# Rank-32 mixing in a fused attention and MLP kernel: the sums of x as six products in 128x64 tiles, and span scores of both tiles ahead of the global ones

## The reference

```
scores = scale * q @ k.T + bias; scores = where(keep, scores, -1e9); a = softmax(scores); x = a @ v
xt = x.transpose(0, 2, 1)
h = xt @ U @ V                       # U: 768 x 32, V: 32 x 768
u = x + h.transpose(0, 2, 1)
u = u + max(u @ w_ch1, 0) @ w_ch2    # 512 -> 2048 -> 512
xk, xr = blends of u and u one position earlier
out = sigmoid(xr @ w_r) * (max(xk @ w_k, 0) ** 2 @ w_v)
```

## Time and profile before

| | |
|---|---|
| median of 3 runs | 524.52 us (522.78 to 524.78) |
| profiled execution, its own time | 522.44 us |
| its span in the trace | 520.7 us |
| PE busy | 508.3 us, 98% |
| DVE, ACT, POOL busy | 184.3, 131.1, 243.4 us |
| PE records in the sums of x (L471) | 192, mean 277 ns |
| granted TensorE clock | 0.999 of full |

### The profile page before, as it was taken

How to read it: one execution, slowest core, us unless ns; L and a number is a source line. 1 busy time by engine, 2 the same in 40 slices (tenths; PEclk the granted TensorE clock), 3 DMA queues, 4 the chain that set the end, 5 groups by cost and what they waited for, 6 DMA issues and landing times.

```text
span 520.7 us, 9725 instructions
## 1 busy us (share of the span) xinstructions
PE 508.3 (98%) x3824; PEld 423.7 (81%) x3824; DVE 184.3 (35%) x479; ACT 131.1 (25%) x352; POOL 243.4 (47%) x228
## 2 busy tenths in 40 slices
PE   4899999999999999999999999999999999999997
PEld 3788888888888888888888888888888888888885
DVE  5777775121313313133131331312443233441323
ACT  4777775101100011000110001121322132213220
POOL 3254657165008100079700729990899579960000
PEclk9999999999999999999999999999999999999999
DMA  6876755204002200024400000000000200020002
GB/s 213 284 242 229 226 189 162 81 0 162 0 0 70 92 0 0 0 66 162 157 20 0 0 0 0 1 0 1 0 1 0 81 0 0 0 81 0 0 0 81
DMA packets 15344, 33.84 MB, mean 65 GB/s; under 512 B 1488, under 2 KB 1872, under 8 KB 15312
## 3 DMA queue, kind: packets, MB, share of 16 engines
q1 hardware_dynamic: 14736, 32.57, 18.5%
q10 hardware_dynamic: 576, 0.84, 0.5%
HBM read 30.25 MB, written 3.15 MB: 64 GB/s over the span
## 4 chain that ended last, share of the span: by engine, by line
PE 97%; DVE 1%; DMA 1%; issue 1%; POOL 0%; ACTq 0%; POOLq 0%
PE psum L582 25%; PE psum L570 25%; PE psum L635 13%; PE psum L626 13%; PE psum L650 6%; PE psum L429 5%; PE psum L441 4%; PE psum L463 3%; PE psum L455 1%; PE psum L471 1%; PE psum L481 1%; PE psum L478 1%; DMA k_in<-in_k 1%; PE psum L479 1%; DVE probs L863 0%
## 5 line engine op out<-in xcount | busy, mean ns | idle before, releaser
L978 DVE SCALAR_TENSOR_TENSOR HL<-psum,HH 128x512 fp32r<-128x512 f32 x48 | 33.2, 692 | 171.9 <-ACT HH L762 171.9
L762 ACT ACTIVATE HH<-psum 128x512 fp32r<-128x512 f32 x48 | 28.8, 600 | 229.3 <-PE psum L570 229.3
L582 PE MATMUL psum<-HH,w2h 128*128 128x512 f32 x192 | 75.0, 391 | 0.0
L570 PE MATMUL psum<-UH,w1h 128*128 (+1 forms) x192 | 74.8, 389 | 0.1
L582 PE MATMUL psum<-HL,w2h 128*128 128x512 f32 x192 | 74.7, 389 | 0.0
L582 PE MATMUL psum<-HH,w2l 128*128 128x512 f32 x192 | 74.7, 389 | 0.0
L570 PE MATMUL psum<-UH,w1l 128*128 (+1 forms) x192 | 74.7, 389 | 0.0
L570 PE MATMUL psum<-UL,w1h 128*128 (+1 forms) x192 | 74.7, 389 | 0.0
L1100 POOL TENSOR_SCALAR w1h<-raw 128x2048 fp32r<-128x2048 f32 x4 | 7.7, 1919 | 118.0 <-PE psum L582 118.0
L1017 DVE TENSOR_TENSOR k_square<-k_relu 128x512 f32<-128x512 f32 x24 | 24.2, 1010 | 66.3 <-ACT k_relu L787 66.2
L681 ACT ACTIVATE probs<-probs,neg_max 128x192 f32<-128x192 f32 x96 | 42.5, 444 | 19.8 <-DVE neg_max L863 19.8
(11 more groups left out here) (118 smaller groups left out, 883.2 us busy)
## 6 DMA issues: line engine op xcount, KB each, us to landing
v_in<-in_v SPq DMA_DIRECT2D x16, 384.0 KB, 4.4
raw<-in_moe_w_ch SPq DMA_DIRECT2D x6, 1024.0 KB, 5.1
v_rest<-in_v_rest SPq DMA_DIRECT2D x8, 384.0 KB, 3.7
out<-result SPq DMA_DIRECT2D x12, 256.0 KB, 2.0
k_in<-in_k SPq DMA_DIRECT2D x7, 432.0 KB, 3.9
q_in<-in_q SPq DMA_DIRECT2D x7, 384.0 KB, 3.1
raw<-in_moe_w_ch SPq DMA_DIRECT2D x8, 256.0 KB, 4.3
raw<-in_moe_w_v SPq DMA_DIRECT2D x2, 1024.0 KB, 5.1
```

Of the source, the lines that this page charges most:

```text
L570: mm = pe.matmul(bank[4 + f % 2][:, 0:BLK], w[:, kt, f * P:(f + 1) * P], x[:, kt, ds(blk * BLK, BLK)], start=kt == 0 and n == 0, stop=kt = ...
L582: mm = pe.matmul(bank[d][:, 0:BLK], w[:, f, d * P:(d + 1) * P], x[:, f % 2, :], start=f == 0 and n == 0, stop=f == FQ - 1 and n == 2)
L762: act.activation(HH[:, f % 2, :], bank[4 + f % 2][:, 0:BLK], ACT.Relu).then_inc(hid_high, 1)
L978: dve.scalar_tensor_tensor(out=HL[:, f % 2, :], in0=bank[4 + f % 2][:, 0:BLK], scalar=0.0, in1=HH[:, f % 2, :].bitcast(F32), op0=ALU.max, ...
```

## The change

`U` is laid out twice side by side (64 columns in place of 32), and its tile moves from beside `x_nat` to behind `probs_t`. The sums of x are six products, one per position tile, each 64 columns wide, in place of twelve that are 32 wide. Even tiles go to partitions 0 to 63, odd tiles to 64 to 127. High and low rows of `A4` now alternate (high 0 to 31 and 64 to 95, low 32 to 63 and 96 to 127), so `a_low` subtracts in two instructions of 32 partitions, and `a_ready` counts to 2 for each pair. V stands four times over as before. In `scores` the loops are exchanged: the span products of both tiles come first, then the global ones.

```diff
@@
-        U = region("U", [P, ST, RANK])
@@
+        U = region("U", [P, ST, 2 * RANK])
@@ def scores(n):
-                for i, t in unit_tiles(n):
-                    for frm, w, to in ((t * P, SPAN, i * (WIN + GLOB)), (None, GLOB, SPAN + i * GLOB)):
+                for w in (SPAN, GLOB):
+                    for i, t in unit_tiles(n):
+                        to = i * (WIN + GLOB) if w == SPAN else SPAN + i * GLOB
                         for j in range(GROUPS):
                             for h in range(2):
                                 r = slice(h * D, (h + 1) * D)
-                                k_at = BAND if frm is None else frm + j * GROUP
+                                k_at = t * P + j * GROUP if w == SPAN else BAND
@@ def sums_of_x(x):
                 for t in range(ST):
-                    for side in (t % 2, t % 2 + 2):
-                        mm = pe.matmul(bank[M_BANK][side * RANK:(side + 1) * RANK, 0:P], U[:, t, :], x(t),
-                                       start=t < 2, stop=t >= ST - 2)
+                    side = t % 2
+                    mm = pe.matmul(bank[M_BANK][side * 2 * RANK:(side + 1) * 2 * RANK, 0:P], U[:, t, :], x(t),
+                                   start=t < 2, stop=t >= ST - 2)
@@ def mixing(p, part):
-                    pe.wait_ge(a_ready, p + 1)
+                    pe.wait_ge(a_ready, 2 * p + 2)
@@ def a_low(p):
-                r = slice(2 * RANK, 4 * RANK)
-                dve.tensor_tensor(A4[r, p % 2, :], bank[M_BANK][r, 0:P], A4[r, p % 2, :].bitcast(F32),
-                                  ALU.subtract).then_inc(a_ready, 1)
+                for side in range(2):
+                    r = slice((2 * side + 1) * RANK, (2 * side + 2) * RANK)
+                    dve.tensor_tensor(A4[r, p % 2, :], bank[M_BANK][r, 0:P], A4[r, p % 2, :].bitcast(F32),
+                                      ALU.subtract).then_inc(a_ready, 1)
```

More of the change, by code:

```diff
@@ L37, in block_kernel @@
     DM = H * D
-    RANK = mix_u.shape[2]
+    RANK = mix_u.shape[2] // 2
     BH = B * H
@@ L1217 @@
     laid["counts"] = laid["counts"].astype(np.int64).view(np.int32)
-    laid["moe_U"] = inputs["moe_U"].reshape(tiles, P, -1).transpose(1, 0, 2)
+    laid["moe_U"] = np.tile(inputs["moe_U"].reshape(tiles, P, -1).transpose(1, 0, 2), (1, 1, 2))
     laid["moe_V"] = np.tile(inputs["moe_V"], (4, 1))
```

## The result

The changed kernel takes 525.35 us (median of 21 executions) against 522.29 us for the kernel before (21 executions): ratio 1.0058, 95% interval 1.0042 to 1.0073, so 3.06 us or 0.58% slower. Measured again, beside other kernels, it was 524.58 against 522.33 us, ratio 1.0040 (1.0018 to 1.0062). Three executions far above all others (639.72 and 979.9 us, with mean granted clocks of 0.758 and 0.895, and 1786.04 us of the kernel before) are in no ratio. The time forecast, 525.4 us, was met, but partly by offset: its base of 523.6 us was 1.3 too high and its step of +1.8 us 0.5 to 1.3 too low. That the time came out to a tenth of a microsecond is luck.

A forecast was written before the change was run, and what follows sets the result against it. In six of eight pairs the path was taken to run from scores through DVE and ACT to a_low and PE's L478, with PE's stream otherwise. 1.92 - 0.10 = +1.8 us on 523.6 gave 525.4 us, range 522.9 to 527.8.

The forecast's parts named there:

- its base of 523.6 us: Time of the kernel before, taken as the mean of the known executions at 522.4, 522.8, 524.5 and 524.8 us.
- its step of +1.8 us: Whole kernel: 1.92 us for the split subtraction less 0.10 us for pair 6.
- The second subtraction: DVE's a_low: second half starts 0.32 us behind the first, on the path in pairs 0 to 5, +1.92 us.
- PE's saving: Sums of x on PE: 0.66 us in place of 0.79, 0.13 us less per pair, hidden in pairs 0 to 5.
- Pair 6: The one pair where PE's shorter sums count, up to the later end of a_low: minus 0.1 us.
- Rival 1: Time lost between PE's shapes is on the path, the second subtraction is not: -0.9 us, 522.7 us, chance 0.08.
- Scores and U: The new score order and the doubled load of U in the fill were each taken as worth 0.
- rival 2: Narrow scores in a row run at 0.03 us each: -2.9, in sum -1.1 us, 522.5 us, chance 0.07.
- rival 3: Narrow scores in a row starve for weights, 0.09 for 0.06 us: in sum +4.7 us, 528.3 us, chance 0.07.
- rival 4: The sums' two 128x64 parts take turns, 1.32 us in place of 0.79: +3.8 us, 527.4 us, chance 0.04.
- rival 5: The subtraction's halves overlap wholly on DVE, a_low ends at most 0.1 us later: +0.5 us, 524.1 us, chance 0.12.
- the forecast's own range of 1.2 to 2.0 us: Range of the slowdown if the forecast itself holds, which was given a chance of 0.62.

The follow-up runs named there:

- run 1: The kernel before with only a_low split into two subtractions of 32 partitions; 526.0 us, ratio 1.0107.
- run 10: The changed kernel with ACT's copy of the sums moved between the two exponents of the first head; 522.17 us, ratio 1.0005.
- run 7: The kernel before with the first half of a pair's mixing placed behind the scores on PE, ACT's copy for it moved likewise; 524.07 us, ratio 1.0019.
- run 8: The changed kernel with one masked subtraction over 128 partitions and the first half of the mixing behind the scores; 523.68 us, ratio 1.0026.
- run 9: The kernel before with ACT's copy of the sums between the two exponents of the first head; 521.73 us, ratio 0.9984.
- run 11: The changed kernel with one masked subtraction over 128 partitions and ACT's copy of the sums between the two exponents; 521.49 us, ratio 0.9987.
- run 3: The changed kernel with the scores in their old order, span and global products alternating by tile; 525.74 us, ratio 1.0061.
- run 2: The kernel before with U laid out twice and moved, the sums still twelve products of 32 columns; 522.17 us, ratio 1.0003.
- run 5: The kernel before with 15 more DVE instructions in the branch that is never taken; 523.55 us, ratio 1.0036.
- run 6: The changed kernel without the subtraction in the branch that is never taken; 523.4 us, ratio 1.0015.
- run 12: The changed kernel itself, measured again beside the early-copy kernels; 524.58 us, ratio 1.0040.
- the masked kernels: The three kernels, run 4, run 8 and run 11, with a_low as one masked subtraction over 128 partitions; ratios 1.0023, 1.0026 and 0.9987.
- run 4: The changed kernel with a_low as one masked subtraction over all 128 partitions; 522.58 us, ratio 1.0023.

## Why the prediction was right, and what it left out

**The second subtraction: right in mechanism and size.** The forecast gave a step of 0.32 us and +1.92 us over six pairs, on the path in full. The step is 0.32 us, the period went from 9.98 to 10.30, and run 1 reproduces this with nothing else changed. Run 10 shows the cause by moving the chain 0.44 us earlier with the same two instructions in place: PE's wait falls to some 0.1 us and the period to 9.86.

**PE's saving: right in sum, wrong in its parts.** The forecast was 0.13 us per pair, as sums of 0.66 us. The sums take 0.71 us (59.06 less 58.35), and L464 gives back the rest: 0.56 us to the transposes (59.62 less 59.06), where L463 took 0.62. Together it is 0.14. That it is hidden in pairs 0 to 5 was right, and runs 7 and 8 and runs 9 and 11 bring it out, 0.14 and 0.13 us. Pair 6, where it was to count by 0.10, gained 0.14: from pair 5's first mixing product to pair 6's is 9.49 us after (90.84 less 81.35) and 9.63 before (86.53 less 76.90). The rule of "TensorEngine Tiling (Array Packing)", Key Properties, in the Trainium skill, that a change of tiling mode drains the engine, agrees with these rows; run 7, with two more changes of mode in a round and 0.33 us more, is the plainest. Rival 1, which put the saving on the path and not the subtraction, fell with the period.

**Scores and U: right.** First score to L456 stayed at 0.80 us and run 3 equals the changed kernel, so rivals 2 and 3 fell; U twice as wide is worth nothing (run 2). The two parts of 128x64 run side by side, so rival 4 fell, and the halves of the subtraction don't overlap, so rival 5 fell.

**What the sum left out is the end of the program.** It took the attention as "the only stage that the change touches", and the tail is 0.9 us longer. With it the sum is 1.92 - 0.13 + 0.92 = +2.7 us, inside both measured intervals (2.2 to 3.8 and 0.9 to 3.2 us), where +1.8 is under the first, and the forecast's own range of 1.2 to 2.0 us holds neither of the measured steps, 3.06 and 2.25. So of the 1.3 us by which the step was too low at the first measurement, 0.9 lie here.

This also moved the result to the edge of what the prediction called telling: slower by over 0.5% had a chance of 0.11, by rivals 3 and 4. The first measurement, 0.58% (0.42 to 0.73), is there by neither of them, and the second, 0.40%, is under it.

The cause of the longer tail is the length of DVE's program, by experiment: 15 unused instructions bring it on (run 5), and leaving 14 out takes it away (run 6). An eleventh instruction packet and the long tail came together in runs 1, 3, 5, 10 and 12, and in the seven others there was neither. How the packet delays the store is seen only in part: it lies at 523.6 to 523.8 us among the last store's packets, and when all others have landed, five packets of that store still come one by one between 524.5 and 524.9, as from one DMA engine that has fallen behind. That last part is a reading, not shown. The Trainium skill ("Runtime: NRT & Kernel Launch", Instruction fetch mechanics) says of crossing a block boundary in the program that its cost is mostly hidden. For DVE itself that holds here (run 5's period stays at 9.98 us); for a store whose landing ends the program it was 0.9 us.

**Do the times bear the sum out?** In part. Executions with a mean granted clock under 0.998 are among the longest (the next paragraph shows where one of them lost its clock), so I leave them out on both sides. The means then differ from the kernel before by 2.6 us in run 12, 0.9 in run 5, 0.1 in run 10 and -0.9 in run 11. Period, pair 6, tail, and the 0.3 us of the masked kernels add up to 2.7, 0.9, 0.1 and -1.0. Runs 1, 4 and 6 fit less well: 3.8 us (four executions) for 2.9, 1.0 for 0.5, and 1.2 for 1.8.

**What stays open: the first 26 us.** In the profiled execution of the changed kernel the first mixing product of pair 0 is at 29.83 us and in run 12 at 28.31, where it was at 26.75; only 0.32 us of that is the subtraction. In eleven of the fourteen traces PE stops between two groups of the same L455 product (L456 after the change), with no releaser: for 1.30 us before, 1.91 after, 2.18 in run 12, and 0.81 to 1.91 in the others. In runs 4, 5 and 9 it doesn't stop. A 16 KB instruction packet of q8 starts 2.2 to 2.5 us ahead of the end of each stop (before: 16.64 and 18.94 us; after: 18.25 and 20.49). In the three traces without a stop it starts 3.1 to 3.6 us ahead of the start of the same product. So a late fetch of PE's program fits all fourteen traces, but no experiment moved the fetch alone. A stop of 0 to 2.2 us is as large as most of what single executions of one kernel differ by; that it is the reason is not shown. In the profiled execution there is something more. Windows of 12 to 20 and 20 to 26 us of it, and 20 to 26 of run 12 (the number behind the last engine is the granted clock):

```profile
12.00:20.00 8.00, 6.07 (x146) 5.27 (x143) 5.54 (x32) 6.60 (x28) 2.66 (x2) 1.00 0.99 333
20.00:26.00 6.00, 5.51 (x101) 4.79 (x101) 2.26 (x12) 2.14 (x10) 0.91 (x1) 0.72 0.38 131
```

```profile
20.00:26.00 6.00, 5.59 (x152) 4.91 (x153) 3.52 (x15) 3.32 (x14) 0.91 (x1) 1.00 0.59 211
```

Behind the stop, from 20.46 us on, PE ran for 3.4 us at 1.2 in place of 2.4 GHz, which makes the mean 0.72; six transposes took 1.54 us, not 0.87. From the product's second part to the next round's L456 it is 3.99 us (24.48 less 20.49), where it was 2.53 before (21.47 less 18.94), so the lower clock cost some 1.5 of the 2.3 us by which this execution is above the median. Runs 3 and 6, with stops of 1.84 and 1.91 us, show the same fall. Run 12 stopped for longer and kept its clock, so the length of the stop alone doesn't decide it. The changed kernel's executions fall apart the same way: four with a mean clock of 0.997 took 527.6 to 527.8 us, fifteen with 0.998 or more took 523.5 to 526.7.

## What to carry to other kernels

Price an edit on the chain that ends last, not on the engine that looks busiest: the saving of 0.13 us per pair was real and hidden, the 0.32 us on a small engine was on the path, and moving one copy by 0.44 us in a third engine's queue took 0.44 us per pair off the changed kernel, more than either. Where an instruction is split, look first for one that does all partitions with a mask: here it cost 0.06 us per pair in place of 0.32. And compare the tail and the count of instruction packets before explaining half a per cent by executed work, since code that never runs can move the end of the program.

## What was not expected of the hardware

- 15 instructions that are never executed lengthened the program's end by 0.9 us (4.2 in place of 3.2), with one 8 KB instruction packet more (11 in place of 10). How the packet holds up the last store is not shown.
- Two subtractions of 32 partitions in disjoint rows don't overlap on DVE: 0.61 us for two of 0.29. Over 128 partitions the masked form takes 0.35.
- One more excursion from 64x64 to 128x128 tiles and back costs PE 0.33 us in a round (run 7).
- The stop of PE in the fill falls at the same instruction, behind 6 of 16 records of L455, in kernels with old and new sums alike. It lasts 0.8 to 2.2 us where it shows, in eleven of fourteen traces, and ends 2.2 to 2.5 us behind the start of a 16 KB instruction packet.
- PE's granted clock fell to half for 3.4 us behind stops of 1.84, 1.91 and 1.91 us (runs 3 and 6, and the changed kernel) and did not behind one of 2.18 us (run 12).
